# Early stages of a fused recurrence and two MLPs: the second unit's mask in two parts and its output by tiles, weight lows and one weight rounding moved behind the first mix, early flags in another PSUM bank, and a key rounding moved in front of a mask

## The chip, the cores and the metric

The kernel runs on one core of one Trainium2 chip. The metric is the device time of one execution in microseconds; less is better.

## The reference, cut to what matters

Batch 2, 8 heads of width 48, 768 steps, model width 384, inner width 1024, all in float32.

```
for t in range(S):                       # recurrence
    y[t]  = r[t] . (state + (u * k[t]) v[t]^T)
    state = w[t] * state + k[t] v[t]^T
x   = y with its heads side by side      # 768 x 384 for each batch
xk  = mu_k * x + (1 - mu_k) * x_prev     # the "mixes", with the step before
xr  = mu_r * x + (1 - mu_r) * x_prev
x2  = sigmoid(xr @ w_r) * (relu(xk @ w_k) ** 2 @ w_v)
h   = gelu(x2 @ w_in);  u, v = halves of h
out = x2 + (u * (w_sg @ layernorm(v) + b_sg)) @ w_out
```

## The kernel before

The 768 steps are cut into 6 chunks of 128. A unit is one chunk of one batch: 12 units, 0 to 11, two for each of the 6 stages of the first MLP (`STAGES`). Units 0 and 1 make stage 0's input; stage s works on the dense products of its own chunk while units 2s+2 and 2s+3 (a and b in the code) are worked out beside them. The second MLP follows when all stages are over.

A unit goes so. VectorE scans the decays forward (`prod`, L1440) and back (`suffix`, L1466), scales keys and queries (`k_in` L1474, `r_in` L1482). TensorE makes the scores (`scores`, L753 for units 0 and 1, L771 for the others) in two banks `ps`; VectorE masks them into `att` (`mask`, L1490 or L1497). GpSimd multiplies r and k (`rkp`, L644), TensorE sums them over each head (`bonus`, L810), and VectorE multiplies the result by v (L1509). TensorE transposes the keys (`keys_by_step`), ScalarE copies them out (`keys`, `k_tok`, L1153), and TensorE adds them to the state (`add_state`, L838). The output is a sum of queries on the state (`from_state`, L859) and scores on values (`from_half`, L883; `from_chunk`, L896, in units 0 and 1). VectorE adds the bonus: the last of four head pairs first (`last_output`, L1545), then the main part (`main_output`, L1555) into `X`. In units 0 and 1 TensorE moves the last pair's rows into the main part (`move_last`, L906); in later units a DMA does it (`hand_on`, L406). `add_on` (L1518) forms z, the state with what was added, and `carry` (L1530) scales it. `from_state` waits for z through `added_read`:

```
eng.wait_ge(z_done, n - N)
```

where n is the number of units carried, so unit 3's `from_state` waits for the z of unit 2.

A mix (6 in a stage: 2 kinds by 3 blocks of 128 rows, the `MIXES`, kind 1 for w_r first) is half on ScalarE (`part_now`, L1180), half on VectorE (`mix_now`, L1564); ScalarE rounds it (`mix_high`, L1190) and VectorE takes the rest (`mix_low`, L1570). Each float32 product is three products of rounded halves: high by high, high by low and low by high. So every weight has a high part rounded by ScalarE (`high_weight`, L1131) and a low part, a difference, made by GpSimd or VectorE (`low_part` L420; `low_half` L427 makes 512 of 1024 columns of one of the three 128-row parts of w_k). The key activations are squared and split the same way: `key_high` on ScalarE (relu L1214, square to `k2_h` L1218, square to `sq` L1222), `key_low` on VectorE for the first two tiles (L1603), on GpSimd for the rest (L669). `key_high` of the third tile waits for the first key low before it writes `sq` again.

All dense products of the first MLP are L928, in three PSUM banks used in turn (`MT` is the order of tiles: r, k, v of each stage, RS, KS and VS; `filled` and `emptied` wait for one).

A flag for each stage tells whether a decay is out of range: ScalarE checks a unit (`check`), TensorE sums (`flag_of`, L819), ScalarE puts it out (`flag_out`, L1171), and SyncE, VectorE and ScalarE wait for it before the stage's mix (`choose`, `chosen`). It lies in the bank of the outputs, in columns which unit b's output overwrites, so `flag_of` waits for unit a's output and `from_state` of unit b for the flag.

The order on each engine is written out by hand; each queue runs in order, and the waits are semaphores. DMA loads of units and weights are issued by SyncE.

## Time and profile before

| | |
|---|---|
| median of 3 runs | 314.63 us (314.49 to 314.73) |
| the profiled execution's own time | 314.62 us |
| its span, first to last instruction | 312.9 us |
| TensorE matmuls busy | 305.7 us, 98% |
| VectorE busy | 202.8 us, 65% |
| ScalarE busy | 157.8 us, 50% |
| GpSimd busy | 112.0 us, 36% |

The span is what the trace holds; 1.7 us lie around it. Busy times overlap. PE is TensorE's matmuls, PEld its weight loads, DVE VectorE, ACT ScalarE, POOL GpSimd, SP SyncE. A matmul's busy time counts its passage through the array, so successive ones overlap.

### The profile page before, as it was taken

What the parts mean: (1) busy time and instruction counts of PE and PEld (TensorE: products, weight loads), DVE (VectorE), ACT (ScalarE), POOL (GpSimd) and SP (SyncE); (2) the same over time, 40 slices, a digit from 0 to 9 for tenths busy, and PEclk for the clock granted to TensorE, in tenths of its full rate; (3) what the DMA queues carried; (4) which work ended last, traced back from release to release, by engine and by line L of the source; (5) the groups of instructions that cost most, each with busy time, mean ns of one, the idle gap of its engine ahead of it and who ended that gap; (6) DMA issues with size and microseconds to landing.
All of it is one profiled execution on the core that took longest, in us unless ns stands there. A gap on an engine that the chain in (4) does not pass through costs nothing.

```text
span 312.9 us, 7312 instructions
## 1 busy us (share of the span) xinstructions
PE 305.7 (98%) x2882; PEld 290.0 (93%) x2882; DVE 202.8 (65%) x349; ACT 157.8 (50%) x323; POOL 112.0 (36%) x107
## 2 busy tenths in 40 slices
PE   8989999999999999999999999999999999999996
PEld 3769889999999999999999998999999989999995
DVE  6989988999897899697152368935437266034332
ACT  6479855853686467467646937552113035311100
POOL 7450340075056506713610504751331048122310
PEclk9999999999999999999999999999999999999999
DMA  7999008107305412300043272000000300000012
GB/s 230 404 393 399 16 17 314 60 2 230 158 2 194 141 55 56 143 6 2 8 148 115 60 258 86 0 2 0 3 0 17 135 0 1 2 0 0 2 50 101
DMA packets 11176, 29.82 MB, mean 95 GB/s; under 512 B 1216, under 2 KB 5888, under 8 KB 9856
## 3 DMA queue, kind: packets, MB, share of 16 engines
q1 hardware_dynamic: 10720, 28.85, 25.5%
q8 instruction: 23, 0.38, 0.5%
q10 hardware_dynamic: 416, 0.45, 0.4%
q14 instruction: 17, 0.14, 0.1%
HBM read 26.45 MB, written 2.36 MB: 92 GB/s over the span
## 4 chain that ended last, share of the span: by engine, by line
PE 87%; DMA 4%; DVE 3%; ACT 2%; SPq 2%; issue 1%; DVEq 0%; ACTq 0%
PE dense L928 36%; PE dense L373 5%; PE dense L371 5%; PE dense L372 5%; DMA wk_raw<-in_moe_w_k 4%; PE puy L373 3%; PE puy L372 3%; PE puy L371 3%; PE ps L371 3%; PE ps L373 3%; PE ps L372 3%; PE puy L883 2%; PE ps L771 2%; PE puy L859 2%; PE pkt L373 2%; PE pkt L371 2%
## 5 line engine op out<-in xcount | busy, mean ns | idle before, releaser
L669 POOL TENSOR_TENSOR k_l<-sq,k_h 128x512 fp32r<-128x512 f32 x22 | 30.4, 1384 | 27.0 <-ACT sq L1222 27.0
L928 PE MATMUL dense<-xkr_h,wk_h 128*128 128x256 f32 x144 | 38.5, 289 | 0.0
L928 PE MATMUL dense<-k_h,wv_h 128*128 128x256 f32 x144 | 38.4, 288 | 0.0
L928 PE MATMUL dense<-k_h,wv_l 128*128 128x256 f32 x144 | 36.5, 283 | 0.0
L928 PE MATMUL dense<-xkr_h,wk_l 128*128 128x256 f32 x144 | 36.2, 283 | 0.0
L928 PE MATMUL dense<-k_l,wv_h 128*128 128x256 f32 x144 | 32.9, 283 | 0.0
L732 POOL TENSOR_TENSOR gated_l<-gf,gated_h 128x384 fp32r<-128x384 f32 x16 | 16.2, 1012 | 46.4 <-ACT gated_h L1370 36.4
L928 PE MATMUL dense<-xkr_l,wk_h 128*128 128x256 f32 x144 | 30.4, 283 | 0.0
L1370 ACT CAST gated_h<-gf 128x384 fp32r<-128x384 f32 x16 | 8.2, 514 | 42.9 <-DVE gf L1766 42.9
L928 PEld LDWEIGHTS dense<-xkr_h,wk_h 128*128 128x128 f32 x144 | 27.5, 191 | 0.3
L928 PEld LDWEIGHTS dense<-k_h,wv_h 128*128 128x128 f32 x144 | 27.0, 191 | 0.4
L928 PEld LDWEIGHTS dense<-xkr_h,wk_l 128*128 128x128 f32 x144 | 26.7, 192 | 0.0
L928 PEld LDWEIGHTS dense<-k_h,wv_l 128*128 128x128 f32 x144 | 26.5, 192 | 0.0
L928 PEld LDWEIGHTS dense<-k_l,wv_h 128*128 128x128 f32 x144 | 24.1, 192 | 0.0
L1180 ACT ACTIVATE xf<-X,par 128x256 f32<-128x256 f32 x36 | 17.6, 505 | 11.3 <-DMA X<-y 11.3
L928 PEld LDWEIGHTS dense<-xkr_l,wk_h 128*128 128x128 f32 x144 | 23.3, 192 | 0.0
L644 POOL TENSOR_TENSOR rkp<-inw 128x512 f32<-128x512 f32 x6 | 7.7, 1288 | 42.6 <-DVE r_in L1482 26.5
L1564 DVE SCALAR_TENSOR_TENSOR xf<-X,omu,xf 128x256 f32<-128x256 f32 x36 | 16.7, 479 | 5.1 <-ACT xf L1180 4.4
L706 POOL TENSOR_TENSOR rstd<-vare,half_neg 128x1 f32<-128x1 f32 x12 | 9.3, 773 | 29.8 <-DVE vare L1744 29.8
L1214 ACT ACTIVATE relu<-dense 128x512 f32<-128x512 f32 x24 | 14.2, 590 | 9.6 <-PE dense L928 9.6
L1190 ACT CAST xkr_h<-xf 128x256 fp32r<-128x256 f32 x36 | 14.3, 398 | 8.8 <-DVE xf L1564 8.8
L653 POOL TENSOR_TENSOR rkp<-inw,par 128x512 f32<-128x512 f32 x6 | 6.2, 1038 | 34.5 <-issue 34.5
(250 smaller groups left out, 917.1 us busy)
## 6 DMA issues: line engine op xcount, KB each, us to landing
inw<-in_units SPq DMA_DIRECT2D x10, 1026.5 KB, 5.0
vb<-in_vT SPq DMA_DIRECT2D x12, 384.0 KB, 7.0
wsg_raw<-in_wsgT SPq DMA_DIRECT2D x1, 2304.0 KB, 10.2
out_y<-y_out SPq DMA_DIRECT2D x12, 192.0 KB, 1.9
wk_raw<-in_moe_w_k SPq DMA_DIRECT2D x3, 512.0 KB, 10.3
wv_raw<-in_moe_w_v SPq DMA_DIRECT2D x4, 384.0 KB, 15.1
win_raw<-in_moe_w_in SPq DMA_DIRECT2D x3, 512.0 KB, 4.7
inw<-in_units SPq DMA_DIRECT2D x2, 512.0 KB, 5.1
```

The costliest lines, as they stand in the source:

```text
L371: pe.matmul(o, a_h, b_h, start=first and n == 0, stop=False, skip_group_check=True)
L372: pe.matmul(o, a_h, b_l, start=False, stop=False, skip_group_check=True)
L373: mm = pe.matmul(o, a_l, b_h, start=False, stop=last and n == len(pairs) - 1, skip_group_check=True)
L669: pool.tensor_tensor(k2_l[:, 2 * n:2 * n + 2], sq[:, j % 2].rearrange("p (g t) -> p g t", g=2), k2_h[:, 2 * n:2 * n + 2], ALU.subtract).th ...
L706: pool.tensor_tensor(rstd[:, t:t + 1], vare[:, t:t + 1], half_neg[:], ALU.pow).then_inc(rstd_done, 1)
L732: pool.tensor_tensor(gated_l[:, x, cols], gf[:, ng % 2], gated_h[:, x, cols], ALU.subtract).then_inc(gl_done, 1)
L928: return pe.matmul(pm[bk][:, n * T:(n + 1) * T], weight[:, t, cols], inputs[:, t], start=first, stop=last, skip_group_check=True)
L1180: act.activation(batches(xf[:, kt, n]), X[:, s % 2, kt, :, 1:C + 1], ACT.Identity, scale=mu[:, n, kt:kt + 1]).then_inc(t_done, 1)
L1190: act.copy(xkr_h[:, n, kt], xf[:, kt, n]).then_inc(xh_done, 1)
L1214: act.activation(relu[:, j % 2], pm[bk][:], ACT.Relu).then_inc(m_free[bk], 1)
L1370: act.copy(gated_h[:, x, cols], gf[:, ng % 2]).then_inc(gh_done, 1)
L1564: dve.scalar_tensor_tensor(out=batches(xf[:, kt, n]), in0=X[:, s % 2, kt, :, 0:C], scalar=omu[:, n, kt:kt + 1], in1=batches(xf[:, kt, n]), ...
```

## The change

- Unit 1's mask is two instructions, the last pair first (`last_att`), then the other three (`att_done`). TensorE does the last pair of unit 1 (`from_chunk(1, last)`) before unit 0's `move_last`.
- Unit 1's main output is three instructions, one for each 128-row block (`first_done`), and ScalarE's first half-mixes wait for their own block.
- ScalarE rounds the third part of w_k behind the mix of stage 0. VectorE makes none of w_k's lows in front of that mix but five behind it; one of them was GpSimd's.
- On VectorE in stage 0, `key_low(0)` goes in front of `mask(2)`, and `mask(3)` in front of `add_on(2)`.
- The flags of stages 1 and 2 lie in the dense bank that the tile VS[1] takes next; `flag_of` waits only for that bank to be empty, VS[1] waits for the flag to be out, and `from_state` doesn't.
- On ScalarE, `keys(b)` goes before `flag_out` in stage 0, and `key_high(s, 3)` before it in stage 1.

```diff
@@ -240,6 +240,8 @@
         def flag_place(s, n):
+            if s in FLAG_APART:
+                return pm[MT.index(("v", s - 1, VS[1][1])) % NM][0:1, 0:n]
             return py[0:1, STATE:STATE + n] if s else pu[0:1, STATE:STATE + n]
@@ -263,6 +265,7 @@
         z_done, state_done, x_in, total_done = sem("z_done"), sem("state_done"), sem("x_in"), sem("total_done")
+        first_done, last_att = sem("first_done"), sem("last_att")
         sq_w, checked, flag_done, chosen = (sem(n) for n in ("sq_w", "checked", "flag_done", "chosen"))
@@ -330,6 +333,9 @@
+        FLAG_APART = (1, 2)
         HANDED = 2
@@ -382,8 +388,9 @@
-        POOL_LOWS = [("wr", 0, 0), ("wk", 0, 0), ("wk", 0, 1)]
-        DVE_LOWS = [("wk", 1, 0), ("wk", 2, 0), ("wk", 1, 1), ("wk", 2, 1)]
+        POOL_LOWS = [("wr", 0, 0), ("wk", 0, 0)]
+        LOW_HALVES = [(1, 0), (2, 0), (0, 1), (1, 1), (2, 1)]
+        DVE_LOWS = [("wk", n, half) for n, half in LOW_HALVES]
         DVE_LOWS += [("wv", n, 0) for n in range(4)] + [("win", n, 0) for n in range(KT)] + [("wout", 0, 0)]
@@ -673,8 +680,7 @@
             low_part(pool, 0, wl_done)
-            for half in range(2):
-                low_half(pool, parts_of("wk")[0], half, wl_done)
+            low_half(pool, parts_of("wk")[0], 0, wl_done)
             pool.wait_ge(sc_mm, 3)
@@ -813,7 +819,9 @@
                 pe.wait_ge(checked, N * (s + 1))
-                if s:
+                if s in FLAG_APART:
+                    emptied(pe, ("k", s - 1, KS[2][1]))
+                elif s:
                     pe.wait_ge(y_done, N * s + 1)
@@ -849,7 +857,7 @@
                 added_read(pe, states(un))
-                if un % N:
+                if un % N and place(un)[0] not in FLAG_APART:
                     pe.wait_ge(flag_done, place(un)[0] + 1)
@@ -886,7 +894,10 @@
                 pe.wait_ge(s_v[un % 3], 16 * (un // 3 + 1))
-                pe.wait_ge(att_done, un + 1)
+                if un == 1 and pairs == last:
+                    pe.wait_ge(last_att, 1)
+                else:
+                    pe.wait_ge(att_done, un + 1)
                 if un == 1:
@@ -912,6 +923,8 @@
                     pe.wait_ge(m_free[bk], use)
+                if (kind, xs) == VS[1] and s + 1 in FLAG_APART:
+                    pe.wait_ge(flag_done, s + 2)
                 if kind == "r" and xs[0] == 0:
@@ -998,8 +1011,8 @@
             bonus(1)
+            from_chunk(1, last, last_mm)
             move_last(0)
-            from_chunk(1, last, last_mm)
             from_chunk(1, main)
@@ -1174,7 +1187,15 @@
                     act.wait_ge(chosen, s + 1)
-                    given(act, s)
+                    if s:
+                        given(act, s)
+                    else:
+                        act.wait_ge(main_done, N - 1)
+                if s == 0 and n == MIXES[0][0]:
+                    if kt == KT - 1:
+                        given(act, s)
+                    else:
+                        act.wait_ge(first_done, kt + 1)
                 if s:
@@ -1250,9 +1271,10 @@
             high_weight(0)
-            for j in wk:
+            for j in wk[:2]:
                 high_weight(j)
             mix(0)
+            high_weight(wk[2])
             for s in range(STAGES):
@@ -1269,8 +1291,8 @@
                     key_high(s, 3)
+                    keys(b)
                     flag_out(s + 1)
-                    keys(b)
                     act.wait_ge(moved_mm, N)
@@ -1285,8 +1307,8 @@
                     keys(b)
+                    key_high(s, 3)
                     flag_out(s + 1)
-                    key_high(s, 3)
                     hand_on(act, b, 1)
@@ -1487,10 +1509,14 @@
                 if un < 2:
-                    dve.copy_predicated(
-                        att0[:, un].rearrange("p h (g t) -> p h g t", g=PAIRS),
-                        upper[:].bitcast(U32).unsqueeze(1).unsqueeze(1).to_broadcast([P, 2, PAIRS, C]),
-                        score_banks(un).rearrange("p h (g t) -> p h g t", g=PAIRS)).then_inc(att_done, 1)
...
+                    for pairs in ((slice(0, PAIRS),), (slice(PAIRS - 1, PAIRS), slice(0, PAIRS - 1)))[un]:
+                        dve.copy_predicated(
+                            att0[:, un].rearrange("p h (g t) -> p h g t", g=PAIRS)[:, :, pairs],
+                            upper[:].bitcast(U32).unsqueeze(1).unsqueeze(1).to_broadcast(
+                                [P, 2, pairs.stop - pairs.start, C]),
+                            score_banks(un).rearrange("p h (g t) -> p h g t", g=PAIRS)[:, :, pairs]).then_inc(
+                                last_att if pairs.start else att_done, 1)
                     return
@@ -1552,6 +1578,12 @@
                     dve.wait_ge(y_mm, un + 1)
+                if un == N - 1:
+                    for kt in range(KT):
+                        cols = slice(kt * C, (kt + 1) * C)
+                        dve.tensor_tensor(X[:, 0, kt, b, 1:C + 1], y_bank(un)[:, cols], inw[:, un, VF][:, cols],
+                                          ALU.add).then_inc(main_done if kt == KT - 1 else first_done, 1)
+                    return
                 dve.tensor_tensor(X[:, s % 2, :, b, 1:C + 1], blocks(y_bank(un))[:, 0:KT],
@@ -1594,8 +1626,6 @@
                     value(s - 1, *VS[1])
-                if s == 0:
-                    low_half(dve, parts_of("wk")[2], 0, wl2_done)
@@ -1635,25 +1665,24 @@
             main_output(1)
-            low_half(dve, parts_of("wk")[1], 0, wl2_done)
             mix(0)
-            for j in parts_of("wk")[1:]:
-                low_half(dve, j, 1, wl2_done)
+            for j, half in LOW_HALVES:
+                low_half(dve, parts_of("wk")[j], half, wl2_done)
             for s in range(STAGES):
...
                     scan_on(b)
+                    key_low(0)
                     mask(a)
-                    key_low(0)
                     scan_back(b)
...
                     output(a)
+                    mask(b)
                     add_on(a)
-                    mask(b)
                     bonus(b)
```

## Rows read from the trace of the kernel before

**Rows 1.** The page, its first part: busy time, share of the span, instructions.

```profile
PE 305.7 (98%) x2882; PEld 290.0 (93%) x2882; DVE 202.8 (65%) x349; ACT 157.8 (50%) x323; POOL 112.0 (36%) x107
```

**Rows 2.** Windows: stretch, length, busy PE, PEld, DVE, ACT, POOL, clock, DMA, GB/s.

```profile
42.00:300.00 258.00, 258.00 (x2429) 250.24 (x2428) 164.15 (x283) 127.04 (x259) 92.66 (x81) 1.00 0.19 67
```

**Rows 3.** Waits of TensorE: total us, times, longest.

```profile
PE dense L928 <- ACT xkr_h L1190: 1.5, 1, 1.5
...
PE puy L819 <- DVE X L1555: 0.5, 1, 0.5
```

**Rows 4.** Timeline of 14 to 21 us: start, length, engine, line, operation, tiles.

```profile
14.60 1.35 DVE L1490 COPY_PREDICATED att<-upper,dense 128x1024 f32<-128x1024 uint32 x1
...
15.83 0.69 DVE L1509 TENSOR_TENSOR inw<-ps,inw 128x512 f32<-128x512 f32 x1
...
16.93 0.29 DVE L1545 TENSOR_TENSOR y<-pkt,inw 128x128 f32<-128x128 f32 x1 [0.42 <-PE pkt L896]
...
17.40 0.94 PE L906 MATMUL puy<-y,moves 128*128 128x128 f32 x6
...
18.21 1.05 ACT L1131 CAST wk_h<-wk_raw 128x1024 fp32r<-128x1024 f32 x1 [0.64 <-DMA wk_raw<-in_moe_w_k]
18.44 0.56 DVE L1555 TENSOR_TENSOR X<-puy,inw 128x384 f32<-128x384 f32 x1 [0.42 <-PE puy L906]
...
18.92 1.24 DVE L427 TENSOR_TENSOR wk_l<-wk_raw,wk_h 128x512 fp32r<-128x512 f32 x1
...
19.16 0.90 ACT L1180 ACTIVATE xf<-X,par 128x256 f32<-128x256 f32 x2
20.08 0.87 DVE L1564 SCALAR_TENSOR_TENSOR xf<-X,omu,xf 128x256 f32<-128x256 f32 x2
```

**Rows 5.** Timeline of VectorE, 25 to 42 us.

```profile
25.36 1.89 DVE L427 TENSOR_TENSOR wk_l<-wk_raw,wk_h 128x512 fp32r<-128x512 f32 x3
27.16 1.23 DVE L1440 TENSOR_TENSOR_SCAN prod<-inw,one 128x516 f32<-128x516 f32 x1
...
30.52 0.68 DVE L1482 TENSOR_TENSOR r_in<-inw,prod 128x512 f32<-128x512 f32 x1
...
31.45 1.22 DVE L1440 TENSOR_TENSOR_SCAN prod<-inw,one 128x516 f32<-128x516 f32 x1
...
32.89 1.07 DVE L1497 COPY_PREDICATED att<-earlier,ps 128x768 f32<-128x768 uint32 x1
33.85 0.86 DVE L1603 TENSOR_TENSOR k_l<-sq,k_h 128x512 fp32r<-128x512 f32 x1
...
37.27 0.69 DVE L1509 TENSOR_TENSOR inw<-pkt,inw 128x512 f32<-128x512 f32 x1
37.88 1.26 DVE L1603 TENSOR_TENSOR k_l<-sq,k_h 128x512 fp32r<-128x512 f32 x1
39.93 0.29 DVE L1545 TENSOR_TENSOR y<-puy,inw 128x128 f32<-128x128 f32 x1 [0.79 <-PE puy L883]
...
40.61 0.41 DVE L1518 TENSOR_TENSOR z<-puy,state 128x256 f32<-128x256 f32 x1
40.94 1.05 DVE L1497 COPY_PREDICATED att<-earlier,ps 128x768 f32<-128x768 uint32 x1
```

**Rows 6.** Timeline of the other engines, 24 to 43 us.

```profile
24.58 0.41 ACT L1190 CAST xkr_h<-xf 128x256 fp32r<-128x256 f32 x1 [0.28 <-DVE xf L1564]
...
31.83 0.90 PE L771 MATMUL ps<-r_in,k_in 64*64 64x128 f32 x32
...
32.85 1.31 POOL L644 TENSOR_TENSOR rkp<-inw 128x512 f32<-128x512 f32 x1 [13.25 <-PE ps L771]
...
34.75 0.63 ACT L1222 ACTIVATE sq<-relu 128x512 f32<-128x512 f32 x1 [1.07 <-DVE k_l L1603]
...
36.11 1.13 PE L810 MATMUL pkt<-rkp,par 128*128 128x128 f32 x8 [0.65 <-ACT k_tok L1153]
...
42.06 0.67 PE L859 MATMUL puy<-r_in,state 64*64 64x128 f32 x16
```

## The prediction

> **What bounds the kernel now.** I read the page first. TensorE is busy for 98% of the span [rows 1], so the end moves only by what moves TensorE. The windows then say where it isn't full: from 42 to 300 us it is busy for all of 258 us, at a granted clock of 1.00 [rows 2]. So whatever is won or lost before 42 us should reach the end one for one, and an edit behind 42 us earns nothing unless it makes a wait. The view of TensorE's waits has few entries behind the warm-up: 1.5 us before the first dense product, 0.65 us in front of unit 2's bonus product, 0.5 us in front of the flag [rows 3, 6]. The chain of waits goes, in that stretch, through the third w_k part's transfer, its rounding, the first mix, then VectorE's lows, scans and first key low, to ScalarE and back to TensorE. The timeline of 14 to 42 us gives the starts I shift below [rows 4 to 6]. The reader is to see there that VectorE has hardly a gap from 20 to 39 us: TensorE's head start is worth only as much as VectorE can follow.
>
> **Unit 1's output and the first mix.** A 128x128 output takes 0.29 us and a product on 128x512 takes 0.69 us, 0.13 us for each 128 columns and 0.16 us fixed. Two mask instructions in place of one add one fixed share. Before, the last pair's output started at 16.93 behind TensorE, though the bonus product (15.83, 0.69 us) was over at 16.52 [rows 4]. TensorE now gets the last pair first, so this output waits only for the product: 15.83 + 0.16 + 0.69 + 0.04 = 16.72, 0.21 us earlier. The moves (17.40) and the main output (18.44) follow, the latter to 18.23. Its three tiles start some 0.21 us apart; the first ends at 18.52, the last at 18.94, against 19.00. ScalarE no longer rounds a w_k part (18.21, 1.05 us) in front of the mix, so its first half-mix starts near 18.6 in place of 19.16 and takes 0.5 us. VectorE no longer makes a low (18.92, 1.24 us) in front. Its first mix starts at 19.17 in place of 20.08, bound by ScalarE's half: 0.91 us earlier. The mixing itself keeps its pace, and the first dense product comes 0.91 us earlier.
>
> **VectorE's five lows.** Behind the mix stood three lows and then unit 2's scan, 25.36 to 27.16, 0.60 us each [rows 5]. Now there are five, 3.0 us, from 24.45. The second needs the third part's rounding. That starts when ScalarE is done with its last mix, 24.99 less 0.91 [rows 6], and takes 1.05 us, to 25.13; the second low would start at 25.05, so this costs up to 0.1 us, and I take 0.04. Unit 2's scan thus starts at 24.45 + 3.00 + 0.04 = 27.49, 0.33 us later than before. The 1.24 us removed in front and the two lows added behind nearly cancel, and what remains is the later start. For TensorE the first lows come in time: its w_k products start near 24.25.
>
> **Unit 2's scores.** They need the queries, which ended at 31.20 [rows 5]; with 0.33 us they end at 31.53, and with 0.12 us to TensorE the scores start at 31.65 in place of 31.83 [rows 6]. Without this wait TensorE would be there at 30.92. Of its 0.91 us head start 0.18 us is left, and it stands 0.7 us in front of the scores, a new entry in the waits.
>
> **Keys rounded in front of mask 2.** ScalarE's square waited for the key low (33.85, 0.86 us) and started at 34.75; TensorE's bonus product followed at 36.11 [rows 5, 6]. Moved in front of the mask, the low takes the mask's place at 32.89 + 0.33. But there GpSimd forms unit 2's products, from 32.67 (32.85 less 0.18) for 1.31 us or more. The low of 33.85 overlapped that by 0.31 us and took 0.86 us where such a form takes 0.69 us; the one of 37.88, wholly beside GpSimd, took 1.26 us. So a microsecond of overlap costs some 0.5 us. The mask, which reads PSUM, ran beside GpSimd before and took 1.07 us, no more than its 1.05 us elsewhere. The end of unit 3's scan (31.45 + 0.33, 1.22 us) is overlapped too: 0.17 us, by the same rate. So the low starts at 33.39; its length is between 0.69 us (no overlap felt) and 1.26 us (all of it). I take 1.15 us, near the upper end, since GpSimd is slowed as well and lasts longer. It ends at 34.54, the square starts at 34.58, 0.17 us earlier than before, and so does the bonus product, 35.94: TensorE's wait there stays. The GPSIMD Engine Reference of the Trainium skill (section Key points) says that GpSimd shares its SBUF interfaces with VectorE and that VectorE instructions with two SBUF inputs contend; the 1.26 us against 0.69 us agree. By that rule the exchange speaks against this edit, since it puts an instruction with two SBUF inputs where one with a PSUM input was.
>
> **Unit 2's output and the early flag.** VectorE is now late by 0.33 + 0.17 us, and by the longer low, 1.15 - 0.86 = 0.29 us: 0.79 us. Unit 2's bonus product on VectorE (37.27) waited for TensorE's 37.24, which absorbs some 0.15 us. The second key low thus goes from 37.88 to 38.5 and ends at 39.76. TensorE's values are 0.17 us earlier, which gives 39.76 for the output's start as well (39.93 before). The flag's 0.5 us wait is gone, since it no longer waits for this output; the product that follows it, 1.1 us, runs before the output is needed. But the queries on the state (42.06 [rows 6]) wait, by the code, for the sum z of unit 2, and the change puts mask 3 in front of that sum. Before, z started 0.68 us behind the output (39.93 to 40.61) [rows 5]. Now the mask stands there (0.96 us to the next start, 32.89 to 33.85): z starts at 39.76 + 0.68 + 0.96 = 41.40 and ends at 41.81. TensorE, without this wait, could be at the queries by some 40.9; it stands until 41.93. Against 42.06 that is 0.13 us won. The flag's gain is turned into a wait for z.
>
> Everything behind is dense [rows 2], and the flag in stage 1, the new order of the keys' rounding and the waits on the flag lie behind work already over: before, TensorE waited for none of them, so they are worth nothing. The gates' later choice costs nothing while the hand-over of units 3 and 5, which comes after it on ScalarE and SyncE, is what the mixing waits for.
>
> **The sum.** In the order in which TensorE meets them: 0.91 us won at the first mix, 0.73 us lost at the scores, 0.01 us more lost at the bonus product, then at most 0.04 us lost between flag and z. That leaves 0.13 us. My rounded lags (0.12 us to TensorE, 0.04 us for the cast) and the near end that I took for the low lean one way, so I put 0.2 us: 314.62 (the profiled execution's own time, span 312.9 and 1.7 us outside it) less 0.2 is 314.4; the median of the runs is 314.63, the same within their spread.
>
> Bounds: with no contention felt by the low and the scan (0.69 us, no 0.17), VectorE is 0.63 us earlier than reckoned and TensorE's bonus product too; 0.13 + 0.63 is about 0.75 us won, 313.9. With the low at 1.26 us, 0.1 us less than reckoned is won, 314.6. The starts of the mix and the lows are good to 0.15 us either way. A difference of 0.2%, 0.63 us, is what a measurement of this kernel tells from no change.
>
> **Rivals.**
> First, no contention: VectorE and GpSimd miss each other, since both starts shift against each other by tenths. It gives 313.9 as worked out. For it: the overlap before was only 0.31 us; against it: GpSimd's start follows the scores, which now come just before VectorE's low. 0.22.
>
> Second, everything shown as a wait is won: head start 0.91, bonus wait 0.65, flag 0.5 us, 2.1 us or 312.5. It needs VectorE to have slack, and [rows 5] show none, and z not to count. 0.05.
>
> Third, the change does nothing that reaches the end: VectorE eats all, 0 to 0.3 us late at z, 314.6 to 314.9. For it: two more lows on the busiest follower; each 0.1 us by which the first mix starts later than 19.17 goes this way. 0.13.
>
> Fourth, slower: the five lows run at the price of the one at 18.92, 1.24 us, which happened beside GpSimd. Five at 1.24 less 0.69 us are 2.75 us more, and unit 2's scores come 2.6 us later than before: 317.2. It decides once the lows together lose more than 0.2 us. Against it: GpSimd has nothing to do from 19.6 to 32.85, and the three lows of 25.36 took 0.63 us each. With smaller forms of it, where the lows or the scan lose a microsecond, 0.10.
>
> **How the numbers follow.** The forecast, 314.4 with its own range of 314.1 to 314.7, has 0.50. Faster by over 0.2% (below 314.0): most of the first rival (0.18), the second (0.05), 0.03 of the forecast: 0.26. Slower by over 0.2% (above 315.26): 0.08 of the fourth, 0.01 of the third and 0.01 of the forecast: 0.10. Within: 0.64. The range takes in the first rival and the third: 313.8 to 314.9, which leaves out the second, the fourth and tails.
>
> **What would show it.** In the profile after: the first dense product near 20.2; a wait of TensorE for r_in before the scores near 31.65; the key low before mask 2 longer than 0.86 us; no wait of the flag, but one of the queries on the state for z near 41.9; and TensorE full behind 42 us. It is wrong if the low takes 0.7 us, if VectorE's scan of unit 2 starts before 27.2, or if a wait turns up behind 42 us.

## The result, and the profile after

The change makes the kernel slower: 315.6 us in the median of 8 runs (315.23 to 315.75) against 314.6 us (314.49 to 315.13, 8 runs), a ratio of 1.0028 with a 95% interval of 1.0017 to 1.0039. The forecast was 314.4 us. The profiled execution took 315.72 us, with a span of 314.0 us at a granted clock of 1.00.

The page's first part, and the windows row of 42 to 300 us:

```profile
PE 305.4 (97%) x2882; PEld 289.8 (92%) x2882; DVE 204.3 (65%) x353; ACT 157.9 (50%) x323; POOL 110.9 (35%) x106
```

```profile
42.00:300.00 258.00, 257.25 (x2422) 249.35 (x2422) 164.79 (x284) 127.02 (x259) 93.07 (x80) 1.00 0.19 67
```

TensorE is busy for 257.25 us where it was for 258.00 [rows 2]; of the missing 0.75 us, 0.58 us is a wait for z, below, and 0.17 us a wait near 147 us. Over the whole it did 305.4 us of work in place of 305.7 [rows 1]. Its waits:

```profile
...
PE dense L941 <- ACT xkr_h L1211: 0.9, 1, 0.9
PE pkt L816 <- ACT k_tok L1166: 0.9, 1, 0.9
PE ps L777 <- issue: 0.8, 2, 0.6
...
PE puy L867 <- DVE z L1544: 0.6, 1, 0.6
```

Against [rows 3]: the wait in front of the first dense product fell from 1.5 to 0.9 us and the flag's is gone. In their place stand 0.8 us at two sets of scores (0.6 us at unit 2's), 0.6 us for z, and the bonus product's wait has grown from 0.65 us [rows 6] to 0.9. Timeline of 15 to 21 us, the counterpart of [rows 4]:

```profile
15.53 0.44 PE L907 MATMUL pkt<-att,vb 128*64 128x128 f32 x4
15.90 0.94 PE L917 MATMUL dense<-y,moves 128*128 128x128 f32 x6
15.93 0.69 DVE L1535 TENSOR_TENSOR inw<-ps,inw 128x512 f32<-128x512 f32 x1
16.65 0.29 DVE L1571 TENSOR_TENSOR y<-pkt,inw 128x128 f32<-128x128 f32 x1
...
17.57 0.94 PE L917 MATMUL puy<-y,moves 128*128 128x128 f32 x6
...
18.61 0.69 DVE L1584 TENSOR_TENSOR X<-puy,inw 128x128 f32<-128x128 f32 x3 [0.87 <-PE puy L917]
...
19.02 0.91 ACT L1201 ACTIVATE xf<-X,par 128x256 f32<-128x256 f32 x2 [1.32 <-DVE X L1584]
...
19.67 0.88 DVE L1596 SCALAR_TENSOR_TENSOR xf<-X,omu,xf 128x256 f32<-128x256 f32 x2 [0.37 <-ACT xf L1201]
```

The last pair's output is early, as forecast (16.65), but TensorE's second moves start at 17.57, later than the 17.40 of before: its row L907 is now cut in two, with the first moves between the parts. The mix starts at 19.67, not at 19.17. VectorE from 25 to 45 us, the counterpart of [rows 5]:

```profile
24.96 3.11 DVE L434 TENSOR_TENSOR wk_l<-wk_raw,wk_h 128x512 fp32r<-128x512 f32 x5
27.99 1.23 DVE L1462 TENSOR_TENSOR_SCAN prod<-inw,one 128x516 f32<-128x516 f32 x1
...
31.35 0.68 DVE L1504 TENSOR_TENSOR r_in<-inw,prod 128x512 f32<-128x512 f32 x1
...
33.63 1.00 DVE L1480 COPY total<-prod 128x4 f32<-128x4 f32 x1
34.55 0.68 DVE L1633 TENSOR_TENSOR k_l<-sq,k_h 128x512 fp32r<-128x512 f32 x1
35.15 1.03 DVE L1523 COPY_PREDICATED att<-earlier,ps 128x768 f32<-128x768 uint32 x1
...
39.14 1.45 DVE L1633 TENSOR_TENSOR k_l<-sq,k_h 128x512 fp32r<-128x512 f32 x1
...
42.13 0.40 DVE L1544 TENSOR_TENSOR z<-puy,state 128x256 f32<-128x256 f32 x1
...
43.05 1.96 DVE L427 TENSOR_TENSOR wv_l<-wv_raw,wv_h 128x768 fp32r<-128x768 f32 x1
44.93 0.28 DVE L1571 TENSOR_TENSOR y<-puy,inw 128x128 f32<-128x128 f32 x1
```

The row to see is the copy of the totals: four elements of each partition take 1.00 us, where the same copy, at 29.35, takes 0.14 us. The other engines, the counterpart of [rows 6]:

```profile
32.13 0.90 PE L777 MATMUL ps<-r_in,k_in 64*64 64x128 f32 x32 [0.63 <-issue]
...
33.16 1.45 POOL L651 TENSOR_TENSOR rkp<-inw 128x512 f32<-128x512 f32 x1 [14.95 <-PE ps L777]
35.26 0.63 ACT L1243 ACTIVATE sq<-relu 128x512 f32<-128x512 f32 x1 [1.53 <-DVE k_l L1633]
...
36.62 1.13 PE L816 MATMUL pkt<-rkp,par 128*128 128x128 f32 x8 [0.86 <-ACT k_tok L1166]
...
38.76 1.28 POOL L651 TENSOR_TENSOR rkp<-inw 128x512 f32<-128x512 f32 x1 [4.16 <-DVE r_in L1504]
...
42.67 0.67 PE L867 MATMUL puy<-r_in,state 64*64 64x128 f32 x16 [0.58 <-DVE z L1544]
```

GpSimd's products run from 33.16 to 34.61, and the copy, begun at 33.63, is over at 34.63. Before, the copy started at 32.81 and took 0.14 us, and GpSimd started at 32.85 [rows 6]: it missed by 0.04 us. The copy's row before, and the one of unit 3's output:

```profile
32.81 0.14 DVE L1458 COPY total<-prod 128x4 f32<-128x4 f32 x1
...
44.30 0.29 DVE L1545 TENSOR_TENSOR y<-puy,inw 128x128 f32<-128x128 f32 x1 [0.25 <-PE puy L883]
```

**Two rulers.** First, VectorE's time from unit 2's queries (r_in, 31.35) to unit 3's output (y, 44.93): 13.58 us after, 13.78 us before (30.52 [rows 5] to 44.30). It leaves out how early an execution reaches the queries, which differs by itself: in six profiles whose kernels have the start of before, it is 30.35 to 30.52 us. Second, the end of the execution less the start of that output: 270.32 us before (314.62 - 44.30). Every experiment below is read by both. In the profiles of 14 of the 20 kernels, before among them, the second ruler lies between 270.31 and 270.40 us, so there the start of VectorE's unit 3 output foretells the end to a tenth of a microsecond. The six others are after (270.79 us), experiments 3 and 6 (270.87 and 270.77), the first kernel of 12 (270.58) and two of experiment 9. Of after's loss 0.63 us are there by 44.93, and some 0.45 us come later, with a hand-over DMA. ScalarE's row of after behind it, and the one of before:

```profile
136.38 0.91 ACT L1201 ACTIVATE xf<-X,par 128x256 f32<-128x256 f32 x2 [2.31 <-DMA X<-y]
```

```profile
134.10 0.91 ACT L1180 ACTIVATE xf<-X,par 128x256 f32<-128x256 f32 x2 [0.68 <-DMA X<-y]
```

After is 0.64 us behind before in ScalarE's rows up to 146 us and 1.09 us from 149.5 us on. Between them lies TensorE's second wait at scores, those of unit 8:

```profile
146.96 0.90 PE L777 MATMUL ps<-r_in,k_in 64*64 64x128 f32 x32 [0.17 <-issue]
```

The late landing goes with the flags. In the profiles of the 13 kernels that have the flags apart, the slower of the two transfers at this place took 3.0 to 3.6 us from issue to landing (after 3.5), and ScalarE waited 1.75 to 2.40 us; in the 7 that don't, before among them, it took 1.9 us, and ScalarE waited 0.68 or 0.69 us. At 3.0 us nothing moves between 146 and 149.5 us; with 3.1 to 3.6 us (six kernels) 0.04 to 0.54 us are lost there. An execution of after without this loss would take 44.93 + 270.32 = 315.25 us; the two fastest took 315.23 and 315.29.

### The profile page after: what moved, and what is told of

Same layout as the page of the kernel before. It is cut to its first block, busy times and chain, and to the rows that moved or that the text cites. A ratio compares the mean times of both kernels' runs of the same rounds, so it can differ in the third digit from the quotient of the medians.

```text
span 314.0 us, 7317 instructions
## 1 busy us (share of the span) xinstructions
PE 305.4 (97%) x2882; PEld 289.8 (92%) x2882; DVE 204.3 (65%) x353; ACT 157.9 (50%) x323; POOL 110.9 (35%) x106
## 4 chain that ended last, share of the span: by engine, by line
PE 89%; DVE 7%; issue 1%; ACT 1%; DMA 1%; DVEq 0%; ACTq 0%
PE dense L941 36%; PE dense L379 5%; PE dense L377 5%; PE dense L378 5%; PE puy L379 3%; PE puy L378 3%; PE puy L377 3%; PE ps L377 3%; PE ps L379 3%; PE ps L378 3%; PE puy L891 2%; PE ps L777 2%; PE puy L867 2%; PE pkt L379 2%; PE pkt L377 2%; PE pkt L378 2%
```

## The experiments

"After" and "before" name the kernel that an edit is made on. All ratios are to before, timed again beside each group of experiments (medians of 314.56 to 314.69 us). "Queries to output" is the first ruler. The code is cut to the lines that matter, "..." marks what is left out.

**1. Is the copy slow because of its form?** The copy with one input becomes a product with two, on after and on before.

```diff
-dve.tensor_copy(total[:, un % 4], prod[:, p, :, C]).then_inc(total_done, 1)
+dve.tensor_tensor(total[:, un % 4], prod[:, p, :, C], one[:, 0:W1 - 1:C + 1],
+              ALU.mult).then_inc(total_done, 1)
```

> The changed kernel, with VectorE's copy of the four totals written as a product with ones (two SBUF inputs in place of one). Theory P (VectorE's single-input copy is held until GpSimd's product of unit 2 is over, 1.00 us in place of 0.14 us): the instruction takes under 0.5 us, the first key low behind it overlaps GpSimd and takes 0.9 to 1.3 us in place of 0.68 us, and of the 0.86 us some 0.3 to 0.5 us is won: 0.3 to 0.5 us less than the changed kernel's 315.3 to 315.7 us. Rival Q (the loss is the order of mask 3 and z together with the late first mix, and the long copy only waits for something that would hold VectorE in any form): no change within 0.1 us, and the product is as long as the copy.

> The kernel before with the copy of totals as a product with ones. Its copies in later units took 0.97 us and 0.78 us, but behind 42 us TensorE waits for nothing: theory P says within 0.1 us of before, since unit 3's copy was over (0.14 us) just before GpSimd's product began. Rival: the late copies do count somewhere, 0.1 us or more is won.

On after 315.24 us (ratio 1.0024, 1.0015 to 1.0033), on before 314.63 us (0.9988, 0.9972 to 1.0004). On after the product also took 1.00 us, at 33.62, and queries to output stayed 13.60 us. The form is not the cause.

**2. GpSimd waits for the copy** (on after).

```diff
 pool.wait_ge(sc_mm, 3)
+pool.wait_ge(total_done, 4)
 products(2)
```

> The changed kernel, with GpSimd's product of unit 2 held until VectorE's fourth copy of totals is done. Theory P: the copy is 0.14 us again, GpSimd's product starts about 0.6 us later, the first key low lies wholly beside it and takes about 1.26 us; net 0.2 to 0.4 us less than the changed kernel. Rival Q: the copy stays long, or the time stays within 0.1 us.

314.69 us (1.0005, 0.9992 to 1.0018): back at before. VectorE and GpSimd from 33.6 us:

```profile
33.65 0.14 DVE L1481 COPY total<-prod 128x4 f32<-128x4 f32 x1
33.70 0.68 DVE L1634 TENSOR_TENSOR k_l<-sq,k_h 128x512 fp32r<-128x512 f32 x1
33.92 1.64 POOL L651 TENSOR_TENSOR rkp<-inw 128x512 f32<-128x512 f32 x1 [15.72 <-DVE total L1481]
```

The copy takes 0.14 us again. Now GpSimd is the one held: its products start inside VectorE's low and take 1.64 us where they take 1.28 us alone. Queries to output is 12.93 us, 0.65 us less than after. The held copy cost that much, which is as much as the 0.63 us that after is late by at unit 3's output.

**3. The key low behind the mask again** (on after).

```diff
-key_low(0)
 mask(a)
+key_low(0)
```

> The changed kernel with the first key low behind mask 2 again. If the low in front of the mask was worth what it seems, ScalarE's square, the key copy and unit 2's bonus product come 0.9 us later while VectorE's own sequence keeps its length: 0.3 to 0.9 us more than the changed kernel. Rival (VectorE's sequence alone sets the end, through z and unit 2's output): no change within 0.1 us.

317.3 us (1.0079, 1.0048 to 1.0109). Queries to output is 14.43 us with the copy still at 1.00 us: this edit of the change was worth 0.85 us even beside the hold. The end is 1.35 us later than 315.25 us even at a clock of 1.00, more than I had expected; the 0.5 us beyond the ruler's 0.85 is the late landing, 3.6 us here. The executions fall into 316.60 to 316.64 us at a clock of 1.00 and 317.96 to 318.27 us at 0.993 or 0.994 (see the last section).

**4. The key low alone, on before.**

```diff
-mask(a)
 key_low(0)
+mask(a)
```

> The kernel before with the first key low in front of mask 2 alone. Theory X (a VectorE instruction with SBUF inputs and one of GpSimd exclude each other: the later one is held until the earlier is over): GpSimd's product starts at about the same moment and first, the low lasts about 1.8 us (held to 34.1, then 0.6 us), the mask and all behind it on VectorE come 1.0 us later, and the time is 0.4 to 1.0 us above before. Rival, the prediction's (each slows the other by half a microsecond for one of overlap): the low takes 1.26 us, the square starts 0.5 us earlier, and the time is within 0.3 us of before.

313.67 us (0.9973, 0.9963 to 0.9984), the lowest median of all (the third kernel of 12 is within 0.1 us of it), where I had expected a loss. By the first ruler 0.86 us of it are the edit's; its profile also reached the queries 0.15 us earlier than before's. VectorE and GpSimd from 32.6 us, and ScalarE's square:

```profile
32.66 0.14 DVE L1458 COPY total<-prod 128x4 f32<-128x4 f32 x1
32.71 1.87 POOL L644 TENSOR_TENSOR rkp<-inw 128x512 f32<-128x512 f32 x1 [13.25 <-PE ps L771]
32.71 0.68 DVE L1603 TENSOR_TENSOR k_l<-sq,k_h 128x512 fp32r<-128x512 f32 x1
...
33.44 0.62 ACT L1222 ACTIVATE sq<-relu 128x512 f32<-128x512 f32 x1
```

The low went first and took its plain 0.68 us; GpSimd took 1.87 us, 1.28 and most of the low's time. ScalarE's square starts 1.31 us earlier than in [rows 6], TensorE's wait for it is gone, and queries to output is 12.92 us. The mask, now behind it, reads PSUM and took 1.07 us beside GpSimd, as before [rows 5]. The low begins with GpSimd or ahead of it, the mask doesn't mind it: the order is better for both.

**5. Z in front of mask 3 again** (on after).

```diff
 output(a)
-mask(b)
 add_on(a)
+mask(b)
```

> The changed kernel with z of unit 2 in front of mask 3 again, as before. Prediction's step (the queries on the state wait for z): z ends 0.95 us earlier, the queries on the state start as soon as TensorE is ready, the scores on values wait for mask 3 instead, and 0.3 to 0.4 us is won. Rival (z is not what TensorE waits for, or mask 3 is as late for the values): nothing is won.

315.29 us (1.0025, 1.0014 to 1.0035), where after's fastest executions are. TensorE's wait for z is gone, but unit 3's output stays at 44.97, for VectorE's w_v low in front of it is held by GpSimd (43.06, 1.99 us), as in after (43.05, 1.96 us). The wait for z was real and cost nothing: in after the held w_v low sets that output, and not TensorE.

**6. The moves first** (on after), which undoes TensorE's new order.

```diff
-from_chunk(1, last, last_mm)
 move_last(0)
+from_chunk(1, last, last_mm)
 from_chunk(1, main)
```

> The changed kernel with TensorE's order of before: unit 0's moves, then unit 1's last pair, then its other pairs; the mask by pairs stays. If the new order costs TensorE a change between kinds of product, unit 1's moves and the first mix come 0.1 to 0.3 us earlier and so does all that VectorE does, 0.1 to 0.3 us less in all. Rival (the order is what brings the last pair's output forward and helps): the first mix comes later, up to 0.2 us more.

315.32 us (1.0019, 1.001 to 1.0028). From the bonus product on VectorE to the mix it is 3.33 us, against 3.74 us after and 4.25 us before, but VectorE's bonus product came later here (16.25), so the mix started at 19.58, 0.09 us earlier. The unit 3 output moved by the same 0.09 us.

**7. One of the two moved lows put back** (on after: GpSimd makes the low of w_k's first part again, VectorE four behind the mix; the low that stood in front of the mix stays behind it).

```diff
-POOL_LOWS = [("wr", 0, 0), ("wk", 0, 0)]
-LOW_HALVES = [(1, 0), (2, 0), (0, 1), (1, 1), (2, 1)]
+POOL_LOWS = [("wr", 0, 0), ("wk", 0, 0), ("wk", 0, 1)]
+LOW_HALVES = [(1, 0), (2, 0), (1, 1), (2, 1)]
...
-low_half(pool, parts_of("wk")[0], 0, wl_done)
+for half in range(2):
+    low_half(pool, parts_of("wk")[0], half, wl_done)
```

> The changed kernel with one of VectorE's five lows given back to GpSimd, four left. Theory P: everything on VectorE from unit 2's scan shifts 0.6 us earlier, and since TensorE waits for the queries, the scores and GpSimd's product shift with it, so the copy is caught again and stays near 1 us; the gain is the 0.6 us, 0.4 to 0.6 us less in all. Rival R (the lows are hidden, the loss lies elsewhere): under 0.2 us.

314.81 us (0.9996, 0.998 to 1.0012). Mix to scan is 7.72 us against 8.32 us after: one low, 0.6 us. The copy is still held (33.11, 1.00 us).

**8. The flags alone, on before**, with the values' bank as in the change and, in stage 0 alone, its order on ScalarE.

```diff
+FLAG_APART = (1, 2)
 ...
-flag_out(s + 1)
 keys(b)
+flag_out(s + 1)
```

> The kernel before with the flags of stages 1 and 2 in the dense bank alone, and the key copy in front of the flag's output. The flag's 0.5 us wait goes; VectorE's z ends at 41.0 and mask 3 at 42.0 us, so the queries on the state start near 41.5 and the scores on values wait for mask 3: 0.3 to 0.45 us less than before. Rival (the gain is given back at mask 3 entirely, or the flag costs something later): within 0.1 us.

314.55 us (0.9986, 0.997 to 1.0003), its lowest 314.12. Queries to output is 13.46 us, 0.32 us less than before; at the end five of the twelve executions show it (314.12 to 314.25), the others lie at 314.45 to 314.92, and the median is not told from before. The transfer near 134 us takes 3.0 us here, 1.9 us in before: the flags alone bring the late landing.

**9. The change mended**: 2, 6 and 7 together on after; then, in a second kernel, 5 as well and all four w_v lows behind unit 3's output; and a third, the latter edit with the flags on before.

```diff
-low_part(dve, wv[0], wl2_done)
 output(b)
-for j in wv[1:]:
+for j in wv:
```

> The changed kernel with three edits: GpSimd's product of unit 2 waits for VectorE's fourth copy of totals, one w_k low is GpSimd's again, TensorE does unit 0's moves first. So far the end followed the start of VectorE's output of unit 3 (the instruction on y) at a distance of 270.3 us in every profile. Theory P' (the loss is VectorE's lateness at that output, made of the held copy, 0.6 us, and of the fifth low, 0.5 us, less what the first mix and the flags win): both gains add, that output starts near 43.9 us, and the time is 314.1 to 314.3 us, 0.3 to 0.5 us below before. Rival (the two runs each removed the same wait, and the gains don't add): 314.6 us.

> The kernel of the run above with z in front of mask 3 again and VectorE's first w_v low behind unit 3's output. With z first TensorE was 0.4 us earlier but VectorE's w_v low, held by GpSimd's product of unit 4, kept unit 3's output from following. Theory: with that low out of the way the 0.2 to 0.4 us are won: 313.8 to 314.0 us. Rival (z's place is worth nothing wherever the low stands, or the low is missed by TensorE): the same as the run above, or later.

> The kernel before with the flags apart, and VectorE's first w_v low behind unit 3's output. The flags alone gave 314.1 to 314.3 us in their better executions, with that output bound by the held low (1.59 us in place of 0.88 us). Theory: the output starts 0.1 to 0.3 us earlier, 313.9 to 314.1 us. Rival (TensorE isn't done earlier than that): no change against the flags alone.

The first: 313.93 us (0.9977, 0.9968 to 0.9987), queries to output 12.92 us. (The 270.3 us that its expectation gives for every profile did not hold for after and experiments 3 and 6.) The second and third brought unit 3's output forward (42.91; 43.77) and were slower than the kernels they were made from (313.93 and 314.55): 314.64 us (0.9998, 0.9985 to 1.001) and 315.36 us (1.0027, 1.0017 to 1.0036). Here the second ruler breaks, 271.40 and 271.20 us. VectorE's row of the second kernel behind that output, and TensorE's at unit 4's scores:

```profile
43.58 3.56 DVE L427 TENSOR_TENSOR wv_l<-wv_raw,wv_h 128x768 fp32r<-128x768 f32 x4
```

```profile
59.42 0.90 PE L779 MATMUL ps<-r_in,k_in 64*64 64x128 f32 x32 [0.27 <-issue]
```

TensorE stands there, and is at 59.42 all the same 0.32 us earlier than in the first mended kernel (59.74). But VectorE's lows end at 47.14, where the first mended kernel's end at 46.94, and its next mix starts at 49.22 in place of 49.03; with some 0.2 us at the late landing (3.3 us) that makes up the profiles' 0.38 us. The third kernel shows it without that: its next mix starts at 50.09, experiment 8's at 49.25, and the profiled executions end 0.85 us apart (314.97 and 314.12). So what carries to the end is VectorE's chain through the next mix to unit 4's queries, and unit 3's output only marks it while the lows around it stay in place.

**10. Key low and flags together, on before.**

> The kernel before with two edits of the change: the first key low in front of mask 2, and the flags' sums in the values' bank. The sum z stays in front of mask 3. Theory A (TensorE's head start counts only as far as VectorE's chain to unit 4's scan is earlier; each edit that brings VectorE's unit 3 output forward brings the end forward as much): the key low was worth 0.9 us, the flags alone 0.5 us at unit 3's output and 0.1 us at the end; both together give unit 3's output near 43.0 us and the end at 313.2 to 313.6. Rival B (the flags' gain is won on TensorE alone and is nothing once VectorE is the later one): the time is that of the key low alone, 313.67, within 0.15 us.

313.9 us (0.9982, 0.9973 to 0.9991), 313.63 the lowest. Unit 3's output is at 43.30 and queries to output 12.92 us, both as with the key low alone (43.29, 12.92): the flags add nothing once VectorE is the later one. That is the rival's mechanism; its time holds for the fastest four (313.63 to 313.71), the median is 0.2 us above it. The rival named 313.67 within 0.15 us, so the median misses it narrowly.

**11. The new start alone, on before**: the split mask, the pair order, the output by tiles, the later rounding and the five lows, without flags, key low and z.

> The kernel before with the new start alone: mask 1 in two, the last pair's output ahead, main output by tiles, the mix before the third w_k part is rounded, five lows behind the mix. No flags, the key low behind mask 2, z in front of mask 3. Theory A (the two moved lows cost VectorE 1.24 us against 0.41 us won at the mix; unit 2's scan starts at 27.99 in place of 27.16, and TensorE meets the scores 0.8 us later while VectorE's whole chain is late): unit 3's output near 45.1 us, the end at 315.2 to 315.6. Rival B (the start is worth nothing and the loss is in the other parts): the time of before, 314.5 to 314.7.

317.68 us (1.0102, 1.0087 to 1.0118). This part alone loses 1.6 us at a clock of 1.00 (316.19 us) and 3.1 us in the four executions at 0.994 or 0.995. Queries to output is 14.40 us: theory A's sum had the late scan but not the hold. VectorE, and ScalarE's square, from 33.7 us:

```profile
33.76 0.99 DVE L1473 COPY total<-prod 128x4 f32<-128x4 f32 x1
34.66 1.05 DVE L1516 COPY_PREDICATED att<-earlier,ps 128x768 f32<-128x768 uint32 x1
35.61 0.67 DVE L1626 TENSOR_TENSOR k_l<-sq,k_h 128x512 fp32r<-128x512 f32 x1
...
36.31 0.63 ACT L1236 ACTIVATE sq<-relu 128x512 f32<-128x512 f32 x1 [2.46 <-DVE k_l L1626]
```

**12. Which half of it.** The first kernel is 6 and 7 on after, without GpSimd's wait; the second before with that start and the key low, without flags; the third the second with GpSimd's wait.

> The change with the two moved lows put back and the moves in front of unit 1's last pair, but without the wait of GpSimd for VectorE's copy of the totals. Theory A (which of VectorE and GpSimd starts first decides 0.9 us: with the lows back, the copy is earlier or later than GpSimd's products by tenths, as in the run with only the lows back, 314.81): 314.4 to 314.9, with a copy of 1.0 us or a held key low in the profile. Rival B (the wait did nothing here): 313.9, as with the wait, with a copy of 0.14 us.

> The kernel before with the start of the change less the two moved lows and with the moves first, and the first key low in front of mask 2; no flags, z in front of mask 3. Theory A (head starts add: the mix is 0.4 to 0.5 us earlier, and the lows take as long as before, so VectorE's whole chain is that much earlier than in the run with the key low alone): unit 3's output near 42.9 us, the end at 313.2 to 313.4, if the copy of the totals stays at 0.14 us; 314.0 if GpSimd holds it. Rival B (the start earns nothing that reaches the end): 313.67 within 0.15 us.

> The kernel of 314.33 us (start of the change less the two moved lows, moves first, key low first, no flags) with GpSimd waiting for the copy of the totals. Theory A (the held copy is worth 0.66 us of VectorE's chain): 12.92 us from unit 2's queries to unit 3's output in place of 13.60, the copy at 0.14 us, the end at 313.6 to 313.75. Rival B (the wait makes GpSimd's products late and TensorE's bonus product with them): 314.0 or more.

314.65 us (1.0004, 0.9995 to 1.0013); 314.33 us (0.9994, 0.9985 to 1.0003); 313.77 us (0.9972, 0.9961 to 0.9983). The copy took 1.00, 1.01 and 0.14 us, and queries to output 13.60, 13.60 and 12.93 us: theory A in the first and, to 0.02 us, the third. In the second it failed: head starts did not add, and the start earned nothing, which is the rival's mechanism; the hold, which the rival left out, put the time 0.66 us above its 313.67. From VectorE's bonus product to unit 2's scan it is 11.33 us, and 11.33 us before. The mix is 0.63 us earlier, and the low that stood in front of it takes 0.62 us behind it. (This ruler is good to some 0.2 us: the first kernel, with the same start, has 11.10 us, the third 11.37.)

**13. A low given to GpSimd** (on before with the key low first and GpSimd's wait): GpSimd makes the low that VectorE made in front of the mix.

```diff
-POOL_LOWS = [("wr", 0, 0), ("wk", 0, 0), ("wk", 0, 1)]
+POOL_LOWS = [("wr", 0, 0), ("wk", 0, 0), ("wk", 1, 0), ("wk", 0, 1)]
...
-low_half(dve, parts_of("wk")[1], 0, wl2_done)
 mix(0)
```

> The kernel before with the first key low in front of mask 2, GpSimd waiting for VectorE's copy of the totals, and VectorE's low in front of the first mix (1.24 us) made by GpSimd between its own two w_k lows. Theory A (VectorE's chain sets the end; GpSimd is idle from 19.6 us on, but holds VectorE's instructions while it works): the mix starts 0.4 to 0.9 us earlier, some 0.5 us are given back where GpSimd's extra low meets the first mixes; unit 2's queries start 0.3 us earlier, near 30.1, then 12.9 us to unit 3's output: 313.3. Rival B (each low on GpSimd costs VectorE as much as it saves, by the holds, or TensorE waits for GpSimd's last low): 313.7 to 314.2.

314.31 us (1.0004, 0.999 to 1.0017). The median is above the rival's range, but it mixes two clocks; the seven executions at 1.00 have a median of 314.19 us, at its upper edge. Theory A failed: the mix starts at 20.12, no earlier than before's 20.08, since it waits for ScalarE's half, and that for a rounding (18.52, 1.05 us). GpSimd's lows last until 20.67 and hold the mix, 1.23 us for two where 0.88 us is plain; TensorE waits 2.1 us for it.

## Why the prediction was wrong, point by point

**What is to be explained.** By its sum the forecast won 0.13 us; without the late landing the change loses 0.63 us. Of the 0.76 us between them the first mix has 0.50 us, a term sized wrongly, and the contention 0.22 us, a mechanism read wrongly. The late landing adds 0.45 us in the profiled execution, and the forecast had it at nothing. The path was wrong too: the forecast followed TensorE to its queries on the state, and what set the end was VectorE's chain (experiments 5 and 9).

**The first mix: failed in size.** "Its first mix starts at 19.17" was 19.67. The removed low and the removed rounding did what was said: VectorE waits 0.37 us for ScalarE's half-mix and for nothing else. But the main output comes at 18.61, not at 18.23, because TensorE's second moves do not gain from the earlier pair: that pair is split off, and the moves behind it start 0.17 us later than before. That is 0.38 us; the other 0.12 us lie between this output and the mix, 1.06 us where the forecast had 0.94. By the trace 0.41 us were won, not 0.91.

**The five lows: right.** They take 3.11 us from 24.96, and the scan starts 0.08 us before their end, so from start to start it is 3.03 us. Predicted were 3.04 us. The scan's start, 27.99 against 27.49, is the missing 0.50 us of the mix and nothing else.

**The scores: right.** They start 0.78 us after the queries' start (31.35 to 32.13), as the 0.80 us of the forecast (their own start is 0.48 us later than forecast, by the mix); "a new entry in the waits" is 0.6 us at that place, for 0.7.

**The key low's contention: the step that failed.** "So a microsecond of overlap costs some 0.5 us" is not how it goes. The one that starts later is held until the other is over, and then takes its whole own time. Worked out from the rows below, its own time then begins some 0.12 us ahead of the other's recorded end. The rows fit: the copy of 33.63 ends at 34.63, its 0.14 us begun at 34.49, GpSimd's products end at 34.61. The second key low (39.14, 1.45 us) ends at 40.59, its own 0.68 us begun at 39.91, GpSimd's products (38.76, 1.28 us) end at 40.04. The low of before, 0.86 us from 33.85, begun in truth at 34.03, with GpSimd until 34.16, had looked like a half rate because the hold was short; the one of 37.88 ended at 39.14, begun at 38.46, with GpSimd's products from 37.32 until 38.60. I had not read that row:

```profile
37.32 1.28 POOL L644 TENSOR_TENSOR rkp<-inw 128x512 f32<-128x512 f32 x1 [3.15 <-DVE r_in L1482]
```

With the rule of halves I priced the low at 1.15 us (it took 0.68) and the scan at 0.17 us (none), and overlooked the four-element copy between them, priced at nothing (it lost 0.86). By the forecast's own starts it was inside: 32.81 + 0.33 = 33.14, with GpSimd from 32.67 for 1.31 us. Before's own trace had such a row: the copy at 67.64 took 0.97 us. The three together are 0.86 - 0.47 - 0.17 = 0.22 us too little.

The page SBUF — State Buffer of the Trainium skill (section SBUF: two separate sides) states this rule: a GpSimd instruction and one of VectorE that runs in a two-port mode, or has two SBUF inputs while GpSimd's reads SBUF, take an exclusive lock, whichever "starts first gets the pair for the whole instruction". The traces agree, with 0.14 against 1.00 us. The prediction had cited the GPSIMD Engine Reference, whose key points say contention without its size.

**Why the copy was caught: TensorE's head start.** GpSimd's products follow the scores' start by 1.03 us, the copy follows the queries' start by 2.28 us. Before, TensorE was busy and took up the scores 1.31 us after the queries' start [rows 5, 6]: GpSimd came at 2.33, just behind the copy. With a head start TensorE waits at the scores, takes them up at 0.78 us, and GpSimd comes at 1.81, 0.47 us ahead of the copy. Experiments 7, 11 and 12 have it whenever TensorE is early, whether GpSimd's low is moved or not (1.81 or 1.82 us in each), and 2, 9 and the third of 12 take it away with one wait. The faster engine released a third, which held the one that sets the end.

**The flag and z: the waits right, their worth not.** The flag's wait is gone, and TensorE stands 0.58 us for z before 42.67. The forecast had 41.93; the difference of 0.74 us is the mix's 0.50 us and the contention's 0.22 us. But z was not what decides (experiment 5), and neither was the flag (10). The forecast put the flags' other effects at nothing, and named a wait behind 42 us as a sign of being wrong: there is one, at 146.96, behind the late landing that goes with the flags.

**The parts in numbers.** The start makes the queries 0.83 us later (30.52 to 31.35): 0.41 us won at the mix, 1.23 us more of lows. From there, with both orders and both states of the copy measured:

| queries to output, us | copy free | copy held |
|---|---|---|
| key low behind the mask | 13.78 (before) | 14.40, 14.43 |
| key low in front | 12.92, 12.93 | 13.58 to 13.60 (after) |

The key low wins 0.80 to 0.86 us and the hold loses 0.62 to 0.68 us, whatever the other does. The flags are not apart in every cell. With the low in front they make no difference (12.92 with and without); with the low behind the mask and the copy free they do, 13.46 us in place of 13.78 (experiment 8), and beside them the low wins only 0.54 us. Left out are the kernels with the w_v low moved (9) and the one profiled at a lower clock (13). The change adds the start's 0.83 us and the hold's 0.66 and takes off the key low's 0.86: 0.63 us, which are 314.62 + 0.63 = 315.25 us in an execution without the late landing. The forecast's fourth rival, slower by lows that run at 1.24 us each, had the sign and not the cause; the first, VectorE and GpSimd missing each other, is the row "copy free" and did not come.

**What stayed open.** The one profile of after puts what lies beyond 315.25 us on the late landing near 136 us, and the 20 profiles put that on the flags' edit. That after's other executions, whose median is 315.6 us, have the same cause is only argued, from times that fall into a lower and an upper group. How the flags' edit delays a transfer, and why one landing takes 3.0 and another 3.6 us, no run shows. Of the start, the split mask, the output by tiles and the later rounding were not run one by one.

## What to carry to other kernels

Where VectorE and GpSimd both work on SBUF, write down for each instruction of one the start and end of the other's, by their new times, and let the later one wait in full, even a copy of four elements (the mask, which reads PSUM, did not wait). Look for such a row in the profile at hand first. Before giving an engine a head start, follow what its earlier product releases. And when a bundle moves little, try its parts alone: here one exchanged pair of lines gave 313.67 us, and the rest took it back and more.

## What the hardware showed that I had not expected

A miss of 0.04 to 0.05 us (copy at 32.81, GpSimd at 32.85) is the difference between 0.14 and 1.00 us. At equal recorded starts (32.71 and 32.71 in experiment 4, 32.72 and 32.72 in 10) VectorE went first. The mask, which reads PSUM, took 1.07 us at 33.31 with GpSimd beside it, and 1.03 us at 35.15 without.

In some executions the clock fell behind a long wait of TensorE near the start. Experiment 13, profiled in such a one, after a wait of 2.1 us before 21.53; windows of 18 to 28 us, the clock in the third column from the end:

```profile
18.00:22.00 4.00, 1.93 (x12) 1.13 (x11) 2.37 (x5) 2.87 (x6) 2.67 (x3) 1.00 1.02 387
22.00:24.00 2.00, 2.00 (x12) 2.00 (x11) 1.66 (x5) 2.00 (x7) 0.00 (x0) 0.52 1.07 378
24.00:26.00 2.00, 2.00 (x13) 2.00 (x13) 1.87 (x6) 1.72 (x5) 0.00 (x0) 0.63 1.08 426
26.00:28.00 2.00, 2.00 (x29) 1.80 (x28) 2.00 (x4) 1.64 (x3) 0.00 (x0) 1.00 1.01 409
```

TensorE ran mostly at the lower of its two levels (1.2 for 2.4 GHz) from 22 to 26 us. The five executions of this kernel at a mean clock of 0.995 took 315.63 to 315.80 us, the seven at 1.00 took 314.15 to 314.38: 1.5 us for one fall. Experiments 3 and 11, with waits of 1.8 us in front of the bonus product, show the same two groups. Before, with 1.5 us of wait, has it rarely: 7 of its 133 executions timed beside the experiments, five of them in one group of 29 (316.37 to 316.50 us at 0.995). In after, with 0.9 us, it was not seen in 8. The profiles of experiments 3 and 11 fell in executions at 1.00, so where their clock fell isn't shown.
